# Attention scores as unsplit row-tiled products, and three expert pieces loaded during attention

## The reference

```python
# 1. attention, q, k, v of 4 batches x 8 heads x 768 x 64
scores = q @ k.T / 8 + bias                   # bias = -slope[head] * distance
keep   = is_global | is_local                 # first 8 keys, or the last 96 up to the query
a      = softmax(where(keep, scores, -1e9))
x      = a @ v                                # -> 3072 tokens x 512
# 2. soft MoE, 8 experts with 4 slots each, phi 512 x 32
logits = x @ phi
slot_in = softmax(logits, axis=0).T @ x       # 32 x 512
slot_out = relu(slot_in @ w1) @ w2            # w1 8 x 512 x 1024, w2 8 x 1024 x 512
x = softmax(logits, axis=1) @ slot_out
# 3. top-1 MoE: every token goes through its best expert, times its gate
```

## Time and profile before

| | us |
|---|---|
| median of 3 runs (450.1 to 451.07) | 450.58 |
| the profiled execution's own time | 450.2 |
| its span in the profile | 448.5 |
| TensorE matmul, busy | 427.3 (95%) |
| TensorE weight load, busy | 357.0 (80%) |
| VectorE | 240.5 (54%) |
| ScalarE | 211.8 (47%) |
| GpSimd | 207.1 (46%) |

### The profile page before, as it was taken

How to read it: one execution, slowest core, us unless ns; L and a number is a source line. 1 busy time by engine, 2 the same in 40 slices (tenths; PEclk the granted TensorE clock), 3 DMA queues, 4 the chain that set the end, 5 groups by cost and what they waited for, 6 DMA issues and landing times.

```text
span 448.5 us, 9336 instructions
## 1 busy us (share of the span) xinstructions
PE 427.3 (95%) x3056; PEld 357.0 (80%) x3057; DVE 240.5 (54%) x788; ACT 211.8 (47%) x417; POOL 207.1 (46%) x172
## 2 busy tenths in 40 slices
PE   8799999999999997998987997999999999999995
PEld 7699999999999997643424884688888888888884
DVE  6566767777677774566300596556332333333344
ACT  2668888787888863431110007264333333232344
POOL 4999888888888810002001007034334344433422
PEclk9989999999999998999999999999999999999999
DMA  7699988976676211999997587511111111111221
GB/s 228 261 417 364 373 343 303 396 259 250 251 261 226 80 54 24 379 385 408 404 387 270 142 304 269 202 37 58 58 58 58 58 58 58 35 58 55 55 54 14
DMA packets 27223, 89.21 MB, mean 199 GB/s; under 512 B 3281, under 2 KB 3281, under 8 KB 27185
## 3 DMA queue, kind: packets, MB, share of 16 engines
q1 hardware_dynamic: 23664, 78.47, 47.1%
q0 software_dynamic: 3360, 9.83, 7.1%
q10 hardware_dynamic: 160, 0.42, 0.5%
HBM read 80.85 MB, written 8.13 MB: 198 GB/s over the span
## 4 chain that ended last, share of the span: by engine, by line
PE 85%; DMA 6%; DVE 4%; POOL 2%; issue 1%; ACT 1%; SPq 0%; ACTq 0%; DVEq 0%; POOLq 0%
PE O L404 16%; PE Yq L1507 11%; PE Yq L1508 11%; PE Yq L1509 11%; PE PT L386 8%; PE S L377 5%; PE S L376 5%; DMA ext<-in_moe_w 4%; PE XTp L819 3%; PE Gp L1445 3%; PE Cp L1418 2%; PE Lp L938 2%; PE Up L828 1%; PE Gp L1480 1%; DMA q_raw<-in_q 1%; PE Sp L1426 1%
## 5 line engine op out<-in xcount | busy, mean ns | idle before, releaser
L461 ACT ACTIVATE shared<-shared,nm 128x256 f32<-128x256 f32 (+1 forms) x192 | 83.8, 484 | 33.1 <-DVE nm L564 33.1
L404 PE MATMUL O<-V,PTs 128*128 128x65 f32 x704 | 90.9, 271 | 0.4 <-ACT PTs L487 0.4
L564 DVE CUSTOM_DVE_ANT_0 shared<-S,TA 128x256 f32<-128x256 f32 (+1 forms) x192 | 68.7, 396 | 37.1 <-PE S L377 34.5
L404 PEld LDWEIGHTS O<-V,PTs 128*128 128x128 f32 x704 | 87.4, 193 | 1.5 <-ACT PTs L487 0.8
L1507 PE MATMUL Yq<-w2h,hh 128*128 x208 | 83.1, 400 | 2.1 <-DVE hl L1806 2.0
L1508 PE MATMUL Yq<-w2l,hh 128*128 x208 | 81.3, 391 | 0.0
L1509 PE MATMUL Yq<-w2h,hl 128*128 x208 | 81.1, 390 | 0.0
L336 POOL TENSOR_TENSOR kl<-k_raw,kh 128x1632 fp32r<-128x1632 f32 x15 | 55.2, 3677 | 9.4 <-ACT kh L471 9.3
L1806 DVE SCALAR_TENSOR_TENSOR hl<-Gp,hh 128x512 fp32r<-128x512 f32 x56 | 38.2, 688 | 39.5 <-ACT hh L1603 37.2
L386 PE MATMUL PT<-ident,shared 128*128 128x128 f32 x352 | 55.4, 276 | 0.1
L376 PE MATMUL S<-kh,qs 128*128 128x256 f32 (+1 forms) x180 | 53.3, 319 | 1.9 <-POOL kl L336 1.9
(11 more groups left out here) (244 smaller groups left out, 569.1 us busy)
## 6 DMA issues: line engine op xcount, KB each, us to landing
mem<-in_moe_w SPq DMA_DIRECT2D x9, 2048.0 KB, 10.6
ext<-in_moe_w SPq DMA_DIRECT2D x6, 2048.0 KB, 19.4
k_raw<-in_k SPq DMA_DIRECT2D x15, 816.0 KB, 7.3
q_raw<-in_q SPq DMA_DIRECT2D x15, 768.0 KB, 5.2
V<-in_v SPq DMA_DIRECT2D x16, 715.0 KB, 4.3
xmem<-in_moe_w SPq DMA_DIRECT2D x2, 2048.0 KB, 10.6
w2l<-in_moe_w SPq DMA_DIRECT2D x2, 2048.0 KB, 13.9
w2h<-in_moe_w SPq DMA_DIRECT2D x1, 2048.0 KB, 7.8
```

Of the source, the lines that this page charges most:

```text
L404: mm = pe.matmul(O[grp % 2][:, at:at + VC], PTs[:, par, (h * kbs + kb) * P:(h * kbs + kb + 1) * P], V[:, buf, h, vb, :], start=(n == 0), s ...
L461: nc.scalar.activation(Pb[:, par, h, 0:width(g)], Pb[:, par, h, 0:width(g)], ACT.Exp, bias=nm[:, par, h:h + 1], scale=-1.0).then_inc(exp_d ...
L564: v.tensor_tensor_reduce(Pb[:, par, h, 0:w], S[par][h][:, 0:w], tab, -SCALE, HUGE, ALU.add, ALU.min, nm[:, par, h:h + 1]).then_inc(biased, 1)
```

## The change

Items 1 to 15 form their scores as item 0 does: the host gives q and k once, head 0 in partitions 0 to 63 and head 1 in 64 to 127, TensorE multiplies them unsplit in two row tiles, and the buffers qs, kh and kl with the work of GpSimd and ScalarE on them are gone. GpSimd only builds the tables of heads 2 to 7, all in one go. Item 0's q and k come in two halves, steps 0 to 2 and 3 to 5. The space freed holds three slots of ext (EARLY = 3), and pieces 4, 5 and 6 are loaded beside items 10, 12 and 14. In the head two casts are gone, the flag is read before the last addition of the distances, ScalarE's exp table is loaded before the flag, phi and w_gate are loaded after it, and there are fewer dummy products.

```diff
@@ TensorE
-        busy(18)
+        busy(14)
...
             if item == 0 and t == 0:
-                pe.wait_ge(first_loaded, 64)
+                pe.wait_ge(first_loaded, 32)
+            elif item == 0 and t == QT // 2:
+                pe.wait_ge(rest_loaded, 32)
             elif t == 0:
-                pe.wait_ge(q_split, item)
-                pe.wait_ge(k_split, item)
+                pe.wait_ge(q_loaded[buf], loads(item))
+                pe.wait_ge(k_loaded[buf], loads(item))
             at, w = ((t - 1) * KSLOT + GK, 2 * P) if t else (0, P)
             for h in range(2):
-                if item == 0:
-                    rows = slice(h * HD, (h + 1) * HD)
-                    mm = pe.matmul(S[par][h][:, 0:w], q_raw[rows, 0, h, t * P:(t + 1) * P],
-                                   k_raw[rows, 0, h, at:at + w], start=True, stop=True)
-                else:
-                    q = qs[:, buf, h, t * P:(t + 1) * P]
-                    pe.matmul(S[par][h][:, 0:w], q, kh[:, buf, h, at:at + w], start=True, stop=False)
-                    mm = pe.matmul(S[par][h][:, 0:w], q, kl[:, buf, h, at:at + w], start=False, stop=True)
+                rows = slice(h * HD, (h + 1) * HD)
+                mm = pe.matmul(S[par][h][:, 0:w], q_raw[rows, buf, t * P:(t + 1) * P],
+                               k_raw[rows, buf, at:at + w], start=True, stop=True)
...
-            busy(8)
+            busy(6)
@@ SyncE
-                    if item == 2:
-                        sp.wait_ge(qk_done, QT)
-                    else:
-                        sp.wait_ge(q_split, item - 2)
-                        sp.wait_ge(k_split, item - 2)
+                    sp.wait_ge(qk_done, (item - 1) * QT)
...
-                if item % 2 == 0 and item // 2 - 1 < MEMW:
-                    load_piece(sp, item // 2 - 1, mem[:, item // 2 - 1, :])
+                if item % 2 == 0 and item // 2 - 1 < MEMW + EARLY:
+                    early_piece(sp, item // 2 - 1)
@@ SyncE, soft MoE
-        for i in range(MEMW, len(PIECES)):
+        for i in range(MEMW + EARLY, len(PIECES)):
@@ ScalarE
+        act.wait_ge(const_ready, 1)
+        nc.scalar.activation(TA[:, 1, 0:1], ones[:, 0:1], ACT.Exp).then_inc(exp_loaded, 1)
...
-                if g % QT == 5 and g // QT + 2 < ITEMS:
-                    round_keys(g // QT + 2, 0)
-                if g % QT == 0 and 0 < g // QT < ITEMS - 1:
-                    round_keys(g // QT + 1, 1)
@@ VectorE
-        step(v.tensor_copy(rel[:, 0:WT], rel_i[:]))
-        step(v.tensor_copy(key[:, 0:WT], key_i[:]))
-        step(v.tensor_scalar(ta[:, 0:WT], rel[:, 0:WT], 0.0, None, ALU.is_lt))
-        step(v.tensor_scalar(tb[:, 0:WT], rel[:, 0:WT], -1.0, None, ALU.mult))
+        v.tensor_scalar(ta[:, 0:WT], rel_i[:], 0.0, None, ALU.is_lt)
+        step(v.tensor_scalar(tb[:, 0:WT], rel_i[:], -1.0, None, ALU.mult))
...
+        v.scalar_tensor_tensor(ND, ND, nf[:, 6:7], ta[:, 0:WT], ALU.min, ALU.mult)
+        n[0] += 1
+        v.scalar_tensor_tensor(tb[:, 0:WT], ta[:, 0:WT], 0.5, tb[:, 0:WT], ALU.is_lt, ALU.mult).then_inc(table_step, 1)
+        dve.wait_ge(flag_ready, 1)
+        fast = dve.value_load(flag[0:1, 0:1], min_val=0, max_val=1)
+        dve.wait_ge(table_step, n[0])
         v.tensor_tensor(ND, ND, tb[:, 0:WT], ALU.add).then_inc(distances_done, 1)
         dve.wait_ge(distances_done, 1)
-        dve.wait_ge(flag_ready, 1)
-        fast = dve.value_load(flag[0:1, 0:1], min_val=0, max_val=1)
```

More of the change, by code:

```diff
@@ L52 @@
 EXT = 8 - MEMW
+EARLY = EXT - 1
 XSLOTS = TT * D // WSIZE
@@ L121, in build @@
         attended = sem("attended")
[L122 removed]
+        attention(nc, ctx, sb, psum, sem, block, attended, mem, ext, X, shared, ident, ones, Rsel, phi_sb, wg_sb, load_piece,
                   sp_passed, const_ready, rsel_ready, small_loaded, q_d, k_d, v_d, n_d, phi_d, wg_d)
[L124 removed]
+        soft_moe(nc, ctx, sb, psum, sem, block, attended, mem, xmem, ext, X, ident, ones, Rsel, phi_sb, load_piece,
                  slot_loaded, rsel_ready, small_loaded, STR, Cn, CT, c_stored, st_out, ct_out, counting, r_iota, lt_done, c_dram)
@@ L129, in build, with attention @@
         both.close()
-def attention(nc, ctx, sb, psum, sem, block, attended, mem, X, shared, ident, ones, Rsel, phi_sb, wg_sb, load_piece,
+def attention(nc, ctx, sb, psum, sem, block, attended, mem, ext, X, shared, ident, ones, Rsel, phi_sb, wg_sb, load_piece,
               sp_passed, const_ready, rsel_ready, small_loaded, q_d, k_d, v_d, n_d, phi_d, wg_d):
     st = ExitStack()
[L142 to L146, removed]
+    q_raw = sb(st, "q_raw", [P, 2, SEQ])
+    k_raw = sb(st, "k_raw", [P, 2, QT * KSLOT])
     V = sb(st, "V", [P, 2, 2, VB, VC])
@@ L218, in loads, with half @@
         return 16 * ((item + 1) // 2)
+    TQ, TK = SEQ // 2, QT // 2 * KSLOT
+    def half(p, size):
+        return slice(p * size, (p + 1) * size)
     def width(g):
@@ L235, in _ @@
         sp.dma_start(nin[:], n_d.partition_broadcast(P)).then_inc(n_loaded, 16)
-        for h in range(2):
-            rows = slice(h * HD, (h + 1) * HD)
-            sp.dma_start(q_raw[rows, 0, h], q_d[0, rows, h * SEQ:(h + 1) * SEQ]).then_inc(first_loaded, 16)
+        sp.dma_start(q_raw[:, 0, half(0, TQ)], q_d[0, :, half(0, TQ)]).then_inc(first_loaded, 16)
         load_v(sp, 0, 0)
-        sp.dma_start(phi_sb[:], phi_d.rearrange("(c p) s -> p c s", p=P)).then_inc(small_loaded, 16)
-        sp.dma_start(wg_sb[:], wg_d.rearrange("(c p) s -> p c s", p=P)).then_inc(small_loaded, 16)
+        sp.dma_start(q_raw[:, 0, half(1, TQ)], q_d[0, :, half(1, TQ)]).then_inc(rest_loaded, 16)
         sp.wait_ge(flag_ready, 1)
@@ L275, in _ @@
             sp.wait_ge(d_normed, ITEMS + 2)
-            for i in range(MEMW):
-                load_piece(sp, i, mem[:, i, :])
+            for i in range(MEMW + EARLY):
+                early_piece(sp, i)
     @block.gpsimd
@@ L310, in _ @@
         with pool.If(fast > 0):
[L311 to L315, removed]
             pool.wait_ge(distances_done, 1)
[L318 to L337, removed]
+            for h in range(2, HEADS):
+                nc.gpsimd.tensor_scalar(TA[:, h, :], ND, 2.0 ** (-8.0 * (h + 1) / HEADS), 1.0 / SCALE,
+                                        ALU.mult, ALU.mult).then_inc(head_table, 1)
         with pool.Else():
-            pool.wait_ge(iota_done, 7)
+            pool.wait_ge(distances_done, 1)
             nc.gpsimd.iota(drel_i, [[1, SEQ]], base=0, channel_multiplier=0).then_inc(d_ready, 1)
@@ L448, in _ @@
     def _(act):
[L449 to L452, removed]
+        act.dma_start(k_raw[:, 0, half(0, TK)], k_d[0, :, half(0, TK)]).then_inc(first_loaded, 16)
+        act.dma_start(k_raw[:, 0, half(1, TK)], k_d[0, :, half(1, TK)]).then_inc(rest_loaded, 16)
+        act.wait_ge(const_ready, 1)
+        nc.scalar.activation(TA[:, 1, 0:1], ones[:, 0:1], ACT.Exp).then_inc(exp_loaded, 1)
         act.wait_ge(flag_ready, 1)
@@ L462, in exps @@
                                      bias=nm[:, par, h:h + 1], scale=-1.0).then_inc(exp_done, 1)
[L464 to L470, removed]
-            nc.scalar.copy(kh[:, buf, h], k_raw[:, buf, h]).then_inc(k_high, 1)
         with act.If(fast > 0):
             act.wait_ge(distances_done, 1)
+            act.wait_ge(exp_loaded, 1)
             nc.scalar.mul(TA[:, 1, :], ND, 2.0 ** (-8.0 * 2 / HEADS) / SCALE).then_inc(tables_built, 1)
@@ L668, in attention, with soft_moe @@
     st.close()
-def soft_moe(nc, ctx, sb, psum, sem, block, attended, mem, xmem, X, ident, ones, Rsel, phi_sb, load_piece,
+def soft_moe(nc, ctx, sb, psum, sem, block, attended, mem, xmem, ext, X, ident, ones, Rsel, phi_sb, load_piece,
              slot_loaded, rsel_ready, small_loaded, STR, Cn, CT, c_stored, st_out, ct_out, counting, r_iota, lt_done, c_dram):
```

55 lines of the change are left out of this document (29 added, 26 removed).

## The result

| | before | after |
|---|---|---|
| median of 4 runs, us | 450.34 (450.07 to 451.07) | 474.53 (472.86 to 476.03) |
| profiled execution, us | 450.2 | 472.86 |
| its span, us | 448.5 | 471.2 |

The ratio is 1.0534, 95% interval 1.0496 to 1.0572: 5.3% slower. The forecast was 473.9, with a range of 469.5 to 478.5.

The account below looks back on a forecast made before the run. TensorE's own pace was taken to bound attention. Attention's shift of +23.7 us, head and item 0 savings included, and -0.3 for the early pieces gave +23.4, 474.0 beside the median; 473.9 was taken, range 469.5 to 478.5.

Parts of the forecast that it names:

- Scores: Attention: a full step with unsplit row-tiled scores takes 2.11 us instead of 1.75, an item 11.79 instead of 9.83.
- narrow block: Attention: the score block of the narrow 128-column step, taken as 0.43 us, with bounds 0.23 and 0.63.
- The stop at item 1: Item 1's first scores: TensorE's 2.06 us wait for the split and the clock fall go, 3.7 us in all.
- key rounding in item 0: Item 0: it delays ScalarE's copy of the turned P before P times V; 0.5 us saved.
- Head: Kernel start: first transposes at 9.3 instead of 10.59, 1.3 us saved, bounds 0.5 and 1.8.
- nin's landing: Kernel start: nin lands 2.9 us after its issue, so nw moves from 4.46 to 3.8 only, 0.66 us saved.
- an item's lead: Attention: the early pieces' transfers are covered, as the queue orders V and q, k an item ahead.
- Three early pieces: Behind attention: loading pieces 4, 5, 6 earlier changes -0.3 us, as xmem is free no earlier; bounds -2.5 and +1.
- start from an empty queue: Piece loads behind xmem's release: the DMA engines, run dry before it, lose 2.2 us in starting again.
- B: Rival, faster: attention's two tiling switches per step cost nothing, an item takes 9.39 us, time 437.6; chance 0.04.
- C: Rival, smaller loss: the three early pieces bring 16.5 us off the 46.17, time 457.4; chance 0.05.
- D: Rival, larger loss: TensorE, drained twice per step, falls to half clock; one fall per item 24 us, time 498; chance 0.06.

Follow-up runs that it names:

- pair: v_first with TensorE's order in pairs of steps (turn, turn, scores, scores, weigh, weigh), halving the changes of tiling: 460.46 us, ratio 1.0208.
- full_rows: v_first with scores multiplied unsplit over all 128 rows, no row tiles, each head getting both heads' sum: median 480.94 us.
- head_only: The kernel before with the head's edits alone, split products kept: 450.39 us, ratio 0.9981.
- no_early: The changed kernel with pieces 4, 5 and 6 loaded after attention again: 475.21 us, ratio 1.0547.
- v_first: The changed kernel with SP issuing V of an item before it waits for the next item's q and k: 473.63 us, ratio 1.0492.

## Why the prediction was right

- **Scores.** The step that decided was reading item 0's block as the price of all: 2.11 us forecast, 2.11 measured, item 11.79 and 11.79. The one estimated part, the narrow block, was put at 0.43 and is 0.43. Fifteen items give 176.9; that attention went at TensorE's pace before and after is what let the sum be made on one engine. pair and full_rows show that the cause was named rightly too: the gaps go with the tiling and count per change.
- **The stop at item 1.** Gone with its clock fall, as said: steps 4 to 10 take 11.79 us where they took 13.54. The key rounding in item 0 was put at 0.5 and gave 0.51 (step 4 at 16.93; 18.11 - 0.67 - 0.51).
- **Head.** 0.67 us and not 1.3, near the lower bound. The term that failed is nin's landing: I took the 2.9 us of the earlier trace rows, and in the changed kernel its packets landed at some 4.5. The casts were not the bound of the head. head_only shows the term as forecast (nin 2.9, nw at 3.83); in all six kernels with only unsplit products, whose first loads are cut otherwise, nin took 3.5 to 3.8 us, and why isn't shown.
- **What was missed.** SP issues q, k and V together in the changed kernel, for V's own event has long passed when it comes to V; in items with a piece V lands up to 7.7 us later and is wanted after 7.1. The prediction said that the queue had an item's lead; V had not. Twice in this execution, +1.3 us.
- **Three early pieces.** Put at -0.3 us and -0.9 between the two profiles, 2.0 against no_early at equal clock. The mechanism held: behind xmem's release the same eight pieces have to come. Off was the start from an empty queue, put at 2.2 us; by the same sum it came to 1.5 (45.25 less 43.7). Against before the fall of the clock at attention's end blurs it: before had one (29.0 us from step 94 to piece 8), after had none (27.5), and while TensorE is slower the transfers go on. At the end of the whole kernel the gain is too small to tell from no_early's median.
- **Sum.** Forecast +23.7 and -0.3; measured +25.6 to step 94 (head 0.6 and V 1.3 more) and -2.9 behind it, of which 1.5 are the clock fall that this execution didn't have. Two misses of opposite sign stand behind the near hit. That the number came so close is in part luck. The changed kernel's run of 476.03 had a mean granted clock of 0.984 against 0.994 in this one, so falls belong to the spread; the run of 474.74 had 0.996, so they are not all of it.
- **Rivals.** B is refuted by the gaps of 0.17 before score blocks, 88 of 88 from 20 us on, C by no_early, D by the clock of 1.00 through attention. One reading in B was off: of item 0's four score blocks behind transposes three have the gap of 0.17 in the kernel before, and the first, at 11.14, which stands behind waits, has 0.12. The conclusion doesn't need it.

## What to carry to other kernels

Before an operation is swapped for another in all iterations, look whether one iteration already does it: its block, with the gaps around it, is the price, and instruction counts are not (four loads each way, 0.46 against 0.63 us, and 0.20 on the neighbour). Where row tiles stand between full-array work, count the changes of tiling and bunch what lies in tiles; halving them gave back 13 of the 23 us here. A transfer moved earlier is worth only what is left of it behind the last event that releases the others' buffers; and on an in-order queue an event that has long passed for one buffer is no lead if another's wait stands ahead of it.

## What the runs showed of the hardware

- A change between 128-row and 64-row work costs TensorE 0.20 us on the way in and about 0.20 on the way out, once per change, however long the blocks are (0.64 against 0.45 for four transposes, 1.08 against 0.90 for eight). The Trainium skill's TensorEngine Tiling, Tiling Modes, has the drain; its size is from these rows.
- Two float32 products of 64 rows stream beside each other: by the differences above, a block of 256 columns takes 0.43 us without its change of tiling, and 0.86 over all rows (full_rows). The gain in streaming is a factor of 2, and two changes ate it.
- TensorE stands 2.2 to 3.1 us at the end of attention in every kernel profiled without dummies there, and the granted clock falls to half behind it in some executions (before, v_first) and not in others (after, no_early). From step 94 to piece 8 the profiles of before and v_first, with a fall, take 1.5 and 3.2 us more than after's without one, which is more than some of the edits weighed here.
